# Attention probabilities kept whole: fp32 products of 64 columns in place of split fp32r products of 128

## Chip, cores and metric

One core of a Trainium2 chip runs the whole program in one launch. The metric is the device time of one execution in microseconds; the kernel before took 707.22 us (median of three runs, 707.11 to 707.36).

## The reference, cut to what matters

The work is an attention block with a mask from clusters, then a token and channel mixing by a Fourier transform with an MLP, then a gated convolution block. The change touches only the last product of the attention.

```python
q, k, v: (2, 8, 768, 64)   # batch, heads, tokens, head size
mask   = q_assign[:, :, :, None] == k_assign[:, :, None, :]
scores = scale * q @ k.T ; scores = where(mask, scores, -1e9) - max
attn   = exp(scores) / (sum(exp(scores)) + 1e-9)
out    = attn @ v                       # then mixing and the two MLP blocks
```

All inputs are fp32, so every product is made either of fp32 operands or of operands split into a high and a low fp32r part.

## The kernel before, in words

The 16 heads (8 heads of 2 batches, number n) run one after the other. A head's 768 query tokens are six tiles t of 128. For each tile:

- `scores` (lines 1327, 1328) writes two PSUM banks of 384 keys each, by two fp32r matmuls per bank.
- `minimum` (line 912, VectorE) takes the row minimum; scores are negated, so it is the maximum.
- `exponent` (line 697, ScalarE) writes the unnormalised probabilities `prob` and their row sums.
- `turn` (line 1338, TensorE) transposes the tile's six blocks of 128x128 into banks 4 and 5, three blocks each; `hf` names the half.
- `store_high` (line 708, ScalarE) writes the fp32r high part of a half into `pt_h`, and `store_low` (line 919, VectorE) the rest, PSUM less the high part, into `pt_l`. Each takes both halves of each tile.
- `values` (line 1352) multiplies half a head (a = 0 or 1, three tiles, 384 columns) by v. For each key block j of six it runs two matmuls, on `pt_h` and on `pt_l`, with the 128 weight columns `v_n[s][:, j, :, :]` = 64 of v's high part beside 64 of its low part. Part 0 has j = 0 to 2, part 1 has j = 3 to 5: six matmuls each.
- `store_o`, `fold_o` (lines 717, 1362) and `store_x` (line 996) add the upper and the lower 64 rows of the result, turn it back, and divide by the row sum.

TensorE's order is written out by hand in `step` and `head`: a step is turn half 0, scores two tiles ahead, turn half 1; between steps stand a part of `values`, a `fold_o`, and every second head the cluster products `dots` (line 1282), else `turn_mask`. `dots` makes four fp32 products of 32 weight columns each over 384 moving columns, in the four column groups of the array. ScalarE and VectorE have `step` and `head` lists of their own in the same order. Turn half hf waits for `store_low` of the same half of the tile before, since banks 4 and 5 are single.

GpSimd splits q, k and the first MLP weights, and in `split_v` (lines 520 to 527) v, from `raw_v`, loaded by SyncE's `load_v` (line 397). SyncE's `serve` waits for that split before it loads the next v.

Of the kernel before, what the change touches and what calls it, by code (L numbers as in the profile page):

```python
# [18 lines left out]
P = 128  # L19
# [4 lines left out]
NT = S // P  # L24
# [23 lines left out]
AHEAD = 1  # L48
W1_AHEAD = 2
# [9 lines left out]
def build(nc, q_t, k_t, v, centroids, w1, w2, w_in, conv_w, w_out, seq_tab, fix_tab, chan_tab, constants, out):  # L59
    main = ExitStack()  # L60
    with main:
# [42 lines left out]
        raw_v = sb(att, "raw_v", [NT * D])  # L104
        q1, k1, q2, k2, v_n = [None] * 2, [None] * 2, [None] * 2, [None] * 2, [None] * 2
        for s in range(2):
            q1[s] = sb(att, f"q1_{s}", [S], F32R)
            k1[s] = sb(att, f"k1_{s}", [S], F32R)
            q2[s] = sb(att, f"q2_{s}", [S], F32R)
            k2[s] = sb(att, f"k2_{s}", [S], F32R)  # L110
            v_n[s] = sb(att, f"v_n{s}", [NT, 2, D], F32R)
            if s == 0:
                mask_n = sb(att, "mask_n", [R, 2, 2 * 2, C])
                mask_r = [sb(att, f"mask_r{j}", [R, P], F32R) for j in range(4)]
        prob = [sb(att, f"prob{s}", [NT, P]) for s in range(2)]
        pt_h = [sb(att, f"pt_h{a}", [NT, HALF], F32R) for a in range(2)]
        pt_l = [sb(att, f"pt_l{a}", [NT, HALF], F32R) for a in range(2)]
# [67 lines left out]
        q_loaded, k_loaded, v_loaded = sem("q_loaded"), sem("k_loaded"), sem("v_loaded")  # L185
# [12 lines left out]
        low_ready = sem("low_ready")  # L198
# [14 lines left out]
        high_ready = sem("high_ready")  # L213
# [6 lines left out]
        v_high, v_split = sem("v_high"), sem("v_split")  # L220
# [165 lines left out]
        def _(sp):  # L386
# [9 lines left out]
            def load_v(i, s):  # L396
                sp.dma_start(raw_v[:, :].rearrange("p (a r d) -> p a r d", a=2, r=R),
                             token_view(v, s, i)).then_inc(v_loaded, 16)

            def serve(i, s, loads=True):  # L400
# [25 lines left out]
                if loads:  # L426
                    sp.wait_ge(v_split, n + 1)
                    load_v(ahead, 1 - s)
# [20 lines left out]
            sp.wait_ge(v_split, 1)  # L449
# [39 lines left out]
        def _(pool):  # L489
# [30 lines left out]
            def split_v(n, s):  # L520
                pool.wait_ge(v_loaded, 16 * n + 16)
                if n >= 2:
                    pool.wait_ge(o_ready, AHEAD + 2 * n - 2)
                raw = raw_v[:, :].rearrange("p (n d) -> p n d", d=D)
                high(v_n[s][:, :, 0, :], raw).then_inc(v_high, 1)
                pool.wait_ge(v_high, n + 1)
                low(v_n[s][:, :, 1, :], raw, as_f32(v_n[s][:, :, 0, :])).then_inc(v_split, 1)

# [67 lines left out]
            split_v(0, 0)  # L596
            scale_q(1)

            for n in range(1, NH):
# [15 lines left out]
                split_v(n, n % 2)  # L615
# [47 lines left out]
        def _(act):  # L663
# [38 lines left out]
            def store_high(n, t, hf):  # L702

                g, a = 6 * n + t, t // R
                act.wait_ge(turn_ready, 2 * g + hf + 1)
                if t % R == 0 and hf == 0 and n:
                    act.wait_ge(o_ready, AHEAD + 2 * n + a - 1)
                nc.scalar.activation(  # L708
                    pt_h[a][:, R * hf:R * hf + R, (t % R) * P:(t % R + 1) * P],
                    ps[:, 4 + hf, 0:HALF].rearrange("p (j c) -> p j c", j=R),  # L710
                    ACT.Copy).then_inc(high_ready, 1)
# [7 lines left out]
            def step(n, s, t, more=True):  # L719
                store_high(n, t, 0)  # L720
# [4 lines left out]
                store_high(n, t, 1)  # L725
# [158 lines left out]
        def _(dve):  # L884
# [116 lines left out]
            def step(n, s, t, more=True):  # L1001

                store_low(n, t, 0)
# [4 lines left out]
                store_low(n, t, 1)  # L1008
# [6 lines left out]
            def head(i, s):  # L1015
# [7 lines left out]
                store_low(n, 5, 0)  # L1023
                denominator(n, s, 0)
                minimum(m, 1 - s, 1)
                store_low(n, 5, 1)
                invert(n, 0)
                store_low(m, 0, 0)
                denominator(n, s, 1)
                minimum(m, 1 - s, 2)  # L1030
                store_low(m, 0, 1)
                invert(n, 1)
                store_x(n, s, 0, i)
                store_low(m, 1, 0)
# [3 lines left out]
                store_low(m, 1, 1)  # L1038
                if dotting:
                    hits(u)  # L1040
                store_low(m, 2, 0)
# [3 lines left out]
                store_low(m, 2, 1)  # L1045
# [5 lines left out]
            def last_head(i, s):  # L1051
# [3 lines left out]
                store_low(n, 5, 0)  # L1055
                denominator(n, s, 0)
                store_low(n, 5, 1)
# [205 lines left out]
        def _(pe):  # L1263
# [67 lines left out]
            def turn(n, t, hf):  # L1331
# [3 lines left out]
                if g:  # L1335
                    pe.wait_ge(low_ready, 2 * g - 1 + hf)
# [424 lines left out]
```

## Time and profile before

| what | value |
|---|---|
| median of three runs | 707.22 us |
| the profiled execution, its own time | 707.65 us |
| its span, first to last instruction | 705.8 us |
| TensorE busy | 694.2 us, 98% |
| VectorE, ScalarE, GpSimd busy | 375.7, 309.5, 254.7 us |
| heads, from the first turn to the last values | about 18 to 264 us |

A busy share says that records lie over the time, not that the array streams at its best: matmuls overlap, and a short wait between two of them can be covered by the record of the one before. The chain of work that ended last shows it better. It gives each piece of work the time from the end of the piece before to its own end, so that a late matmul group shows as a longer piece. The view by stretches gives busy times in a part of the span.

### The profile page before, as it was taken

The page shows a single profiled execution, that of the slowest core. Times are in us where ns is not written, and L with a number is a line of the kernel's source. Part 1 is how long each engine was busy: PE and PEld are TensorE (multiplying, and loading weights), DVE is VectorE, ACT ScalarE, POOL GpSimd, SP SyncE. Part 2 cuts the span into 40 slices and gives each one's busy share as a digit, 9 for nine tenths or more (in the row PEclk, how much of TensorE's full clock was granted, in tenths as well). Part 3 has the DMA queues.
Part 4 walks back from the last instruction along what each step waited for, and adds up shares of the span by engine and source line. Part 5 has one row for each costly group of instructions (what it writes and reads, how often), then busy time and mean ns, then how long its engine had stood idle before and what let it go on. Part 6 is the DMA issues. An engine that isn't in the chain of part 4 may idle for free.

```text
span 705.8 us, 10209 instructions
## 1 busy us (share of the span) xinstructions
PE 694.2 (98%) x3810; PEld 607.6 (86%) x3810; DVE 375.7 (53%) x710; ACT 309.5 (44%) x634; POOL 254.7 (36%) x280
## 2 busy tenths in 40 slices
PE   8899999999999999999999999999999999999998
PEld 7699889899999999888888888888888899988876
DVE  4898988979888856953113211131111489933410
ACT  4777777777778851311111111121111377743411
POOL 6756896696499132388600000000050070000000
PEclk7899999999999999999999999999999999999999
DMA  5453424434245021143200000010050520000011
GB/s 170 132 134 103 122 78 130 136 81 114 63 130 162 19 66 33 31 120 107 72 1 0 1 1 0 1 60 1 1 178 1 159 80 1 1 31 30 31 46 45
DMA packets 25921, 47.11 MB, mean 67 GB/s; under 512 B 3728, under 2 KB 10768, under 8 KB 25616
## 3 DMA queue, kind: packets, MB, share of 16 engines
q1 hardware_dynamic: 23392, 38.11, 19.2%
q0 software_dynamic: 2336, 7.95, 3.5%
q8 instruction: 31, 0.51, 0.3%
q10 hardware_dynamic: 144, 0.39, 0.2%
q14 instruction: 18, 0.15, 0.1%
HBM read 36.02 MB, written 3.15 MB: 55 GB/s over the span
## 4 chain that ended last, share of the span: by engine, by line
PE 92%; DVE 6%; ACT 1%; issue 1%; POOL 0%; DVEq 0%; ACTq 0%; POOLq 0%
PE ps L1590 19%; PE ps L1556 19%; PE ps L1352 10%; PE ps L1338 10%; PE ps L1638 9%; PE ps L1652 9%; PE ps L1327 5%; PE ps L1328 5%; PE ps L1362 3%; PE ps L1433 2%; PE ps L1282 1%; PE ps L1403 1%; PE ps L1488 1%; DVE pt_l L919 1%; PE ps L1575 1%
## 5 line engine op out<-in xcount | busy, mean ns | idle before, releaser
L1160 DVE SCALAR_TENSOR_TENSOR hid_l<-ps,hid_h 128x512 fp32r<-128x512 f32 x48 | 33.2, 692 | 197.1 <-ACT hid_h L806 197.1
L806 ACT ACTIVATE hid_h<-ps 128x512 fp32r<-128x512 f32 x48 | 28.8, 599 | 223.6 <-PE ps L1556 223.6
L919 DVE TENSOR_TENSOR pt_l<-ps,pt_h 128x384 fp32r<-128x384 f32 x192 | 106.0, 552 | 36.3 <-ACT pt_h L708 35.9
L708 ACT ACTIVATE pt_h<-ps 128x384 fp32r<-128x384 f32 x192 | 94.6, 494 | 37.0 <-PE ps L1338 36.8
L1338 PE MATMUL ps<-cst,prob 128*128 128x128 f32 x576 | 97.3, 278 | 2.3 <-DVE pt_l L919 1.2
L912 DVE TENSOR_REDUCE row_min<-ps 128x1 f32<-128x768 f32 x96 | 91.2, 950 | 2.3 <-PE ps L1328 2.3
L1338 PEld LDWEIGHTS ps<-cst,prob 128*128 128x128 f32 x576 | 69.3, 142 | 21.9 <-issue 14.3
L697 ACT ACTIVATE prob<-ps,row_min 128x768 f32<-128x768 f32 x96 | 86.5, 901 | 2.4 <-DVE row_min L912 2.4
L1590 PE MATMUL ps<-w_h,hid_h 128*128 128x512 f32 x192 | 76.2, 397 | 0.0
L1590 PE MATMUL ps<-w_h,hid_l 128*128 128x512 f32 x192 | 75.5, 393 | 0.0
L1590 PE MATMUL ps<-w_l,hid_h 128*128 128x512 f32 x192 | 74.7, 389 | 0.0
L1327 PE MATMUL ps<-k,q 80*128 80x384 f32 x192 | 74.2, 386 | 0.3 <-issue 0.3
L1352 PE MATMUL ps<-pt_h,v_n 128*128 128x384 f32 x192 | 69.9, 364 | 0.7 <-DVE x L996 0.7
L1328 PE MATMUL ps<-k,q 128*128 128x384 f32 x192 | 66.5, 346 | 0.0
L1352 PE MATMUL ps<-pt_l,v_n 128*128 128x384 f32 x192 | 64.7, 337 | 0.0
L643 POOL DMA_DIRECT2D in_h<-in_moe_w_in x4 | 2.2, 561 | 162.8 <-PE ps L1556 162.8
L1221 DVE SCALAR_TENSOR_TENSOR gate<-act_s,taps,gate 128x768 f32<-128x768 f32 x32 | 36.0, 1125 | 34.3 <-ACT gate L843 33.8
L1638 PE MATMUL ps<-xt_h,in_h 128*128 128x384 f32 x128 | 43.6, 341 | 0.0
L1590 PEld LDWEIGHTS ps<-w_h,hid_l 128*128 128x128 f32 x192 | 36.0, 188 | 8.5
L1638 PE MATMUL ps<-xt_l,in_h 128*128 128x384 f32 x128 | 43.2, 338 | 0.0
L1638 PE MATMUL ps<-xt_h,in_l 128*128 128x384 f32 x128 | 43.2, 338 | 0.0
L1590 PEld LDWEIGHTS ps<-w_l,hid_h 128*128 128x128 f32 x192 | 36.1, 188 | 7.9
(179 smaller groups left out, 1515.0 us busy)
## 6 DMA issues: line engine op xcount, KB each, us to landing
w_raw<-in_moe_w_ch SPq DMA_DIRECT2D x24, 256.0 KB, 2.5
raw_d<-in_q SPq DMA_DIRECT2D x8, 384.0 KB, 3.3
raw_v<-in_v SPq DMA_DIRECT2D x16, 192.0 KB, 2.5
out<-out_s SPq DMA_DIRECT2D x12, 256.0 KB, 2.0
raw_qk<-in_k SPq DMA_DIRECT2D x15, 192.0 KB, 3.3
raw_qk<-in_q SPq DMA_DIRECT2D x15, 192.0 KB, 3.2
q<-q SPq DMA_DIRECT2D x15, 192.0 KB, 3.9
k<-k SPq DMA_DIRECT2D x15, 192.0 KB, 3.4
```

Source lines behind the costliest of these rows:

```text
L697: nc.scalar.activation(prob[t % 2][:, :, :].rearrange("p (h j) c -> p h (j c)", h=2), ps[:, 2 * (t % 2):2 * (t % 2) + 2, 0:HALF], ACT.Exp, ...
L708: nc.scalar.activation(pt_h[a][:, R * hf:R * hf + R, (t % R) * P:(t % R + 1) * P], ps[:, 4 + hf, 0:HALF].rearrange("p (j c) -> p j c", j=R ...
L912: nc.vector.tensor_reduce(row_min[:, col:col + 1], ps[:, 2 * (t % 2):2 * (t % 2) + 2, 0:HALF], axis=AX.XY, op=ALU.min).then_inc(min_ready, 1)
L919: nc.vector.tensor_tensor(pt_l[a][part], ps[:, 4 + hf, 0:HALF].rearrange("p (j c) -> p j c", j=R), as_f32(pt_h[a][part]), ALU.subtract).th ...
L1327: nc.tensor.matmul(bank, q2[s][0:D + C, cols], k2[s][0:D + C, keys], start=True, stop=False)
L1328: last = nc.tensor.matmul(bank, q1[s][:, cols], k1[s][:, keys], start=False, stop=True)
L1338: last = nc.tensor.transpose(ps[:, 4 + hf, j * P:(j + 1) * P], prob[t % 2][:, R * hf + j, :], ident)
L1352: last = nc.tensor.matmul(ps[:, o_bank(n, a), 0:HALF], v_n[s][:, j, :, :], src[:, j, :], start=j == 0 and src is pt_h[a], stop=j == NT - 1 ...
L1556: last = nc.tensor.matmul(ps[:, hid_bank(blk, f), :], st[:, kt, :], mv[:, kt, :], start=kt == 0 and m == 0, stop=kt == KT - 1 and m == 2)
L1590: last = nc.tensor.matmul(ps[:, 4 + j, :], st[f % 2][:, toks], mv[:, f, :], start=f == 0 and n == 0, stop=f == FT - 1 and n == 2)
L1638: last = nc.tensor.matmul(bank, st[:, kt, cols], mv[:, kt, toks], start=kt == 0 and m == 0, stop=kt == KT - 1 and m == 2)
L1652: last = nc.tensor.matmul(ps[:, 6 + n % 2, :], st[:, f, toks], mv[:, f, :], start=f == 0 and m == 0, stop=f == FT2 - 1 and m == 2)
```

## The change

- `pt_h`, `pt_l` become `pt[n % 2][a]`, one fp32 copy of each turned tile, double over the heads. ScalarE's `store_left` copies the left half (bank 4), VectorE's `store_right` the right one (bank 5): one copy of 128x384 per engine and tile where there were two.
- v isn't split. SyncE loads it straight into one of three fp32 buffers, after the head that used the buffer before has finished its products. GpSimd's `split_v` is gone.
- `values` makes one fp32 product per key block, of 64 weight columns over 384 moving ones. Even j go to array columns and PSUM partitions 0 to 63, odd j to 64 to 127; the fold after it is as before and now adds even and odd blocks. Part 0 has four products, part 1 two.
- TensorE's `step` runs the scores first and then both turn halves; the other engines' lists follow.

```diff
+V_BUFS = 3
-        pt_h = [sb(att, f"pt_h{a}", [NT, HALF], F32R) for a in range(2)]
-        pt_l = [sb(att, f"pt_l{a}", [NT, HALF], F32R) for a in range(2)]
+        pt = [[sb(att, f"pt{par}{a}", [NT, HALF]) for a in range(2)] for par in range(2)]
+        v_n = [sb(att, f"v_n{j}", [NT, D]) for j in range(V_BUFS)]
...
             def load_v(i, s):
-                sp.dma_start(raw_v[:, :].rearrange("p (a r d) -> p a r d", a=2, r=R),
-                             token_view(v, s, i)).then_inc(v_loaded, 16)
+                n = 2 * i + s
+                if n >= V_BUFS:
+                    sp.wait_ge(o_ready, AHEAD + 2 * (n - V_BUFS) + 2)
+                sp.dma_start(v_n[n % V_BUFS][:, :, :].rearrange("p (a r) d -> p a r d", a=2),
+                             token_view(v, s, i)).then_inc(v_loaded[n % V_BUFS], 16)
...
                 if loads:
-                    sp.wait_ge(v_split, n + 1)
                     load_v(ahead, 1 - s)
...
-            def store_high(n, t, hf):
+            def store_left(n, t):
                 g, a = 6 * n + t, t // R
-                act.wait_ge(turn_ready, 2 * g + hf + 1)
-                if t % R == 0 and hf == 0 and n:
-                    act.wait_ge(o_ready, AHEAD + 2 * n + a - 1)
+                act.wait_ge(turn_ready, 2 * g + 1)
+                if t % R == 0 and n >= 2:
+                    act.wait_ge(o_ready, AHEAD + 2 * (n - 2) + a + 1)
                 nc.scalar.activation(
-                    pt_h[a][:, R * hf:R * hf + R, (t % R) * P:(t % R + 1) * P],
-                    ps[:, 4 + hf, 0:HALF].rearrange("p (j c) -> p j c", j=R),
-                    ACT.Copy).then_inc(high_ready, 1)
+                    pt[n % 2][a][:, 0:R, (t % R) * P:(t % R + 1) * P],
+                    ps[:, 4, 0:HALF].rearrange("p (j c) -> p j c", j=R),
+                    ACT.Copy).then_inc(left_stored, 1)
...
             def step(n, s, t, more=True):
-                store_high(n, t, 0)
                 if t < 5:
                     exponent(n, s, t + 1)
                 elif more:
                     exponent(n + 1, 1 - s, 0)
-                store_high(n, t, 1)
+                store_left(n, t)
...
-            def store_low(n, t, hf):
+            def store_right(n, t):
                 g, a = 6 * n + t, t // R
-                dve.wait_ge(high_ready, 2 * g + hf + 1)
-                part = (slice(None), slice(R * hf, R * hf + R), slice((t % R) * P, (t % R + 1) * P))
-                nc.vector.tensor_tensor(pt_l[a][part], ps[:, 4 + hf, 0:HALF].rearrange("p (j c) -> p j c", j=R),
-                                        as_f32(pt_h[a][part]), ALU.subtract).then_inc(low_ready, 1)
+                dve.wait_ge(turn_ready, 2 * g + 2)
+                if t % R == 0 and n >= 2:
+                    dve.wait_ge(o_ready, AHEAD + 2 * (n - 2) + a + 1)
+                nc.vector.tensor_copy(pt[n % 2][a][:, R:2 * R, (t % R) * P:(t % R + 1) * P],
+                                      ps[:, 5, 0:HALF].rearrange("p (j c) -> p j c", j=R)).then_inc(right_stored, 1)
...
                 if g:
-                    pe.wait_ge(low_ready, 2 * g - 1 + hf)
+                    pe.wait_ge((left_stored, right_stored)[hf], g)
...
                 if part == 0:
-                    pe.wait_ge(low_ready, 12 * n + 6 * a + 6)
-                    pe.wait_ge(v_split, n + 1)
+                    for stored in (left_stored, right_stored):
+                        pe.wait_ge(stored, 6 * n + 3 * a + 3)
+                    pe.wait_ge(v_loaded[n % V_BUFS], 16 * (n // V_BUFS + 1))
                     if 2 * n + a:
                         pe.wait_ge(x_stored, AHEAD + 2 * n + a - (o_bank(n, a) == 7))
-                for j in range(R * part, R * part + R):
-                    for src in (pt_h[a], pt_l[a]):
-                        last = nc.tensor.matmul(ps[:, o_bank(n, a), 0:HALF], v_n[s][:, j, :, :], src[:, j, :],
-                                                start=j == 0 and src is pt_h[a],
-                                                stop=j == NT - 1 and src is pt_l[a])
+                for j in ((0, 1, 2, 3), (4, 5))[part]:
+                    at = D * (j % 2)
+                    last = nc.tensor.matmul(ps[at:at + D, o_bank(n, a), 0:HALF], v_n[n % V_BUFS][:, j, :],
+                                            pt[n % 2][a][:, j, :], start=j < 2, stop=j >= NT - 2)
...
             def step(n, s, t):
 
-                turn(n, t, 0)
                 if t < 4:
                     scores(n, s, t + 2)
                 else:
                     scores(n + 1, 1 - s, t - 4)
+                turn(n, t, 0)
                 turn(n, t, 1)
```

## Rows read from the trace of the kernel before

**Rows 1.** The page: busy time by engine, and TensorE's granted clock in 40 slices.
```profile
PE 694.2 (98%) x3810; PEld 607.6 (86%) x3810; DVE 375.7 (53%) x710; ACT 309.5 (44%) x634; POOL 254.7 (36%) x280
...
PEclk7899999999999999999999999999999999999999
```

**Rows 2.** The page: the chain that ended last, by engine and by line.
```profile
PE 92%; DVE 6%; ACT 1%; issue 1%; POOL 0%; DVEq 0%; ACTq 0%; POOLq 0%
PE ps L1590 19%; PE ps L1556 19%; PE ps L1352 10%; PE ps L1338 10%; PE ps L1638 9%; PE ps L1652 9%; PE ps L1327 5%; PE ps L1328 5%; PE ps L1362 3%; PE ps L1433 2%; PE ps L1282 1%; PE ps L1403 1%; PE ps L1488 1%; DVE pt_l L919 1%; PE ps L1575 1%
```

**Rows 3.** Busy time by stretch: length, engines, granted clock, DMA share, GB/s.
```profile
42.00:252.00 210.00, 209.08 (x1428) 191.40 (x1427) 180.86 (x373) 164.72 (x378) 145.12 (x166) 1.00 0.39 104
17.00:42.00 25.00, 23.04 (x144) 18.72 (x137) 21.21 (x42) 19.17 (x44) 16.11 (x17) 0.91 0.43 121
```

**Rows 4.** Groups by line and form, 100 to 180 us: busy, mean ns, idle before.
```profile
L919 DVE TENSOR_TENSOR pt_l<-ps,pt_h 128x384 fp32r<-128x384 f32 x64 | 35.3, 552 | 10.4 <-ACT pt_h L708 10.3
...
L708 ACT ACTIVATE pt_h<-ps 128x384 fp32r<-128x384 f32 x64 | 31.6, 493 | 12.6 <-PE ps L1338 12.6
L912 DVE TENSOR_REDUCE row_min<-ps 128x1 f32<-128x768 f32 x32 | 30.4, 950 | 0.0
L697 ACT ACTIVATE prob<-ps,row_min 128x768 f32<-128x768 f32 x32 | 28.8, 901 | 0.0
...
L697 ACT ACTIVATION_READ_ACCUMULATOR prob<-ps,row_min 128x1 f32 x31 | 6.4, 206 | 0.0
```

**Rows 5.** The chain in order of time, 95.2 to 125.7 us: start, length, what.
```profile
98.00 0.33 PE ps L1338 x3
...
101.47 0.44 PE ps L1338 x3
...
103.99 0.12 issue
104.11 0.52 PE ps L1338 x3
...
105.58 0.21 PE ps L1327
...
106.36 0.52 PE ps L1338 x3
106.89 1.06 PE ps L1352 x6
...
120.38 0.27 PE ps L1327
```

**Rows 6.** The chain in order of time, 229.9 to 258.5 us, heads without dots.
```profile
233.01 0.46 PE ps L1338 x3
```

**Rows 7.** The chain in order of time, 10 to 42 us: dots and the turn behind.
```profile
34.17 0.78 PE ps L1282 x8
34.95 0.48 PE ps L1338 x3
```

**Rows 8.** Line 1282, 124.80 to 125.20 us: ns min/median/max, first and last start.
```profile
L1282 PEld LDWEIGHTS ps<-raw_d,cen_b x8: 106/108/109, 124.9 to 125.0; 128*32 128x32 f32 x8
L1282 PE MATMUL ps<-raw_d,cen_b x4: 510/510/510, 124.9 to 124.9; 128*32 128x384 f32 x4
```

**Rows 9.** The chain in order of time, 10 to 42 us: the first head.
```profile
19.29 0.56 DVE pt_l L919
...
28.14 0.57 DVE pt_l L919
```

**Rows 10.** The chain in order of time, 229.9 to 258.5 us: the last head.
```profile
252.54 0.74 DVE row_min L912
...
254.28 1.31 PE ps L1352 x6
```

**Rows 11.** SyncE's queue, 0 to 262 us: who it waited for, total, times, longest.
```profile
SPq L397 <- POOL v_n L497: 95.6, 15, 9.6
```

More of the change, by code:

```diff
@@ L103, in build @@
         raw_qk = sb(att, "raw_qk", [S])
-        raw_v = sb(att, "raw_v", [NT * D])
-        q1, k1, q2, k2, v_n = [None] * 2, [None] * 2, [None] * 2, [None] * 2, [None] * 2
+        q1, k1, q2, k2 = [None] * 2, [None] * 2, [None] * 2, [None] * 2
         for s in range(2):
@@ L110, in build @@
             k2[s] = sb(att, f"k2_{s}", [S], F32R)
-            v_n[s] = sb(att, f"v_n{s}", [NT, 2, D], F32R)
             if s == 0:
@@ L184, in build @@
         cst_loaded, cen_loaded = sem("cst_loaded"), sem("cen_loaded")
-        q_loaded, k_loaded, v_loaded = sem("q_loaded"), sem("k_loaded"), sem("v_loaded")
+        q_loaded, k_loaded = sem("q_loaded"), sem("k_loaded")
+        v_loaded = [sem(f"v_loaded{j}") for j in range(V_BUFS)]
         q2_copied = [sem(f"q2_copied{s}") for s in range(2)]
@@ L197, in build @@
         min_ready = sem("min_ready")
-        low_ready = sem("low_ready")
+        right_stored = sem("right_stored")
         x_stored = sem("x_stored")
@@ L212, in build @@
         exp_ready = sem("exp_ready")
-        high_ready = sem("high_ready")
+        left_stored = sem("left_stored")
         o_stored = sem("o_stored")
@@ L219, in build @@
         q_split, k_split = sem("q_split"), sem("k_split")
-        v_high, v_split = sem("v_high"), sem("v_split")
         cen_cleared = sem("cen_cleared")
@@ L448, in _ @@
             sp.dma_start(stage[:, 0, 0], w1[0, :, :]).then_inc(w1_raw_loaded[0], 16)
-            sp.wait_ge(v_split, 1)
             load_v(0, 1)
@@ L518, in split_qk @@
                 pool.wait_ge(k_split, n + 1)
[L520 to L527, printed above, removed]
             def split_w1(f):
@@ L595, in _ @@
             pool.wait_ge(k_split, 1)
-            split_v(0, 0)
             scale_q(1)
@@ L614, in _ @@
                     split_w1(n)
-                split_v(n, n % 2)
                 if n in (12, 13):
@@ L1001, in step @@
             def step(n, s, t, more=True):
-                store_low(n, t, 0)
                 if t < 4:
@@ L1007, in step @@
                     minimum(n + 1, 1 - s, t - 4)
-                store_low(n, t, 1)
+                store_right(n, t)
             def z_low_part(b, m):
@@ L1022, in head @@
                 step(n, s, 4)
-                store_low(n, 5, 0)
                 denominator(n, s, 0)
                 minimum(m, 1 - s, 1)
-                store_low(n, 5, 1)
                 invert(n, 0)
-                store_low(m, 0, 0)
+                store_right(n, 5)
                 denominator(n, s, 1)
                 minimum(m, 1 - s, 2)
-                store_low(m, 0, 1)
                 invert(n, 1)
+                store_right(m, 0)
                 store_x(n, s, 0, i)
-                store_low(m, 1, 0)
                 if dotting:
@@ L1037, in head @@
                 minimum(m, 1 - s, 3)
-                store_low(m, 1, 1)
                 if dotting:
                     hits(u)
-                store_low(m, 2, 0)
+                store_right(m, 1)
                 if dotting:
@@ L1044, in head @@
                 minimum(m, 1 - s, 4)
-                store_low(m, 2, 1)
+                store_right(m, 2)
                 if dotting:
@@ L1054, in last_head @@
                 step(n, s, 4, more=False)
-                store_low(n, 5, 0)
                 denominator(n, s, 0)
-                store_low(n, 5, 1)
+                store_right(n, 5)
                 invert(n, 0)
```

## The prediction, as written before the result

> **What bounds the kernel now.** I read first the page's busy times. TensorE has records over 98% of the span, and from slice 3 on its granted clock is at the top of its two levels, 2.4 GHz [rows 1]; no other engine passes 53%. Then the chain of work that ended last: TensorE holds 92% of it, and the edited product, line 1352, holds 10% of the span, as does the turn, line 1338 [rows 2]. The view by stretches says where the change can act. From 42 to 252 us TensorE is covered for 209.1 of 210 us, while VectorE (180.9) and ScalarE (164.7) are busy but not full [rows 3]. So an engine that is relieved gives nothing by being relieved; it gives back only the short waits that it causes on TensorE. What counts is the time that TensorE's own pieces take, plus those waits. Both are read from the chain in order of time, since a piece there runs from the end of the one before to its own end.
>
> **Waits that can go.** A turn half (three transposes) takes 0.33 us where nothing holds it up; in the same two heads others take 0.44, 0.12 + 0.52, and 0.52 [rows 5]. The steps behind them all wait for `store_low` of the tile before, that is for a chain turn, store_high (493 ns), store_low (552 ns) with a minimum of 950 ns or an exponent of 901 ns in between [rows 4]. I added what TensorE's pieces in the 30 us of that double head have over their usual length, without the piece behind dots: 0.11, 0.31 and 0.19 from the rows just named, 0.05 of issue ahead of the last, and seven smaller extras that make 0.67, the first a score matmul of 0.21 and the last one of 0.27 where 0.18 is usual: 1.3 us. Such a double head repeats from 42 to about 206 us, 5.4 times: 7.1 us. In the heads without dots the largest extra is 0.13 [rows 6], and all make about 0.2 us per head, four times: 0.8 us. Together 7.9 us.
>
> After the change ScalarE has per tile 901 + 206 (reading the sum) + 493 = 1.6 us and VectorE 950 + at most 552 = 1.5 us [rows 4], against steps of some 2.5 us (15 us a head, six steps). Turn half 0 of the next tile needs `store_left`, which has the second turn half, the values or fold, and the next scores (four matmuls, 0.7 us) to hide behind, about 1.8 us against 0.6. I take all 7.9 us as gained, and keep a third of it as uncertain.
>
> **The first head.** From 19 to 28.8 us the chain runs over VectorE: minima, cluster steps, and seven `pt_l` pieces of 0.46 to 0.57 us, 3.5 us in all [rows 9]. Four right copies take the place of eight low ones, so about 1.5 us of that chain goes; clock and cluster steps stay (the granted clock is 0.91 from 17 to 42 us [rows 3], and a TensorE kept fuller may hold it up, or the scores ahead of the turns may cost some of it back). I take -1.5, between -2.5 and 0. **The last head.** values waits for `store_x` of the head before, behind a minimum and a low store on VectorE: 1.31 us where six matmuls take 1.06, after 3 us of chain on other engines, the 0.74 us minimum among them [rows 5, 10]. One low store fewer (0.55): -0.6.
>
> **What the products cost.** Before: 1.06 us per part [rows 5], 2.11 per half head. After, nothing here has 64 columns, and the nearest rows are those of dots: four fp32 products of 32 columns over 384, one in each column group. Each makes two passes: the eight matmuls start in two bunches, the first four all at 124.9 us [rows 8], and all eight take 0.78 us [rows 7]. So column groups run side by side, each with its own moving columns. A pass over 384 fp32 columns is 0.33 us, by the three transposes of 128 columns in one 0.33 us turn half [rows 5]; hence dots is two passes, 0.65, and 0.12 us of entry. The turn half behind it takes 0.48 in place of 0.33 [rows 7]: 0.15 us of exit. I read both as what it costs to change between a whole array and column groups, since values and turns change into one another at no such price.
>
> Part 0 has four products, two per group, four passes deep: 0.12 + 4 x 0.325 = 1.42. Part 1 has two passes: 0.78. With two exits 2.50 us against 2.11: +0.39 a half head, 32 times, +12.5. Behind seven parts dots follows, in column groups too, and the last two parts stand together: -1.3. Weights of 64 columns load longer than those of 32 (106 ns [rows 8]), the third and fourth pass of a group need a weight load that dots never shows, and the exit now leads into a score matmul with its 128-column weights: 0 to 0.1 us for each of 63 sections, I take 0.035, +2.3. Sum for the products: **+13.5 us**, from +9 to +18. The streaming alone would have been a gain: six passes are 1.95 us against 2.11. The price is the 63 changes.
>
> On this the Trainium skill says, in "TensorEngine Tiling (Array Packing)", Key Properties, that a change of tiling mode drains the engine, though tiles within one mode run side by side. By that rule, the trace agrees: 0.12 + 0.15 us at dots.
>
> **The rest.** GpSimd loses 16 splits of v; TensorE doesn't wait for GpSimd, so nothing. SyncE waited 95.6 us for them at the v load [rows 11], and now waits there for o of head n - 2, the product that those splits waited for themselves: never later than before, so loads and `load_dots` behind it in the queue come no later. v's bytes and descriptors are the same. Everything after 264 us shifts as a whole.
>
> **Sum.** 707.65 (the profiled execution, 705.8 span and 1.85 around it) + 13.5 - 7.9 - 1.5 - 0.6 = 711.15; the profiled execution is 0.43 above the median, so 710.7 us, 0.5% slower. A measurement here tells about 0.2% (1.4 us) from no change.
>
> **Rivals.**
> 1. *The passes queue up.* Matmuls are issued product by product, first pass, second pass; if a second pass that waits for its own group also holds up the other group, one pass (0.33) is lost in each of 63 sections, +20: 731 us. Against: four first passes at 124.9 us. If the column groups didn't overlap at all, six more passes per half head, 32 x 1.95 = +62: about 773. Rows 7 and 8 speak against both, for 32 columns. The Trainium skill, in "TensorE: Matmul & The Clock Gate", Part 3, says that matmuls start and end strictly in program order. By that rule the first of these would come true; whether the bunches of rows 8 are out of program order the trace can't tell.
> 2. *Changing the groups is cheap* (the other side): the 0.27 us at dots belong to its own waits (mask_stored, raw_d) and not to the array. Then the products cost 12.5 - 63 x 0.27 and the 2.3 less, about -4 and with the waits -14: 693 us. Half that price gives 702. It decides where a change in and out costs under about 0.21 us (0.27 - 3.5/63). For it: dots waits on two semaphores. Against: values and turns wait too and pay nothing, and the turn behind dots pays as well.
> 3. *The waits stay*: `store_left` stands behind the exponent of the next tile; if that is late, the 7.9 us come back in part: 715 to 719.
> 4. *Both sides cancel*: changes at 0.2 us rather than 0.3, 705.8 to 708.6.
>
> **Chances.** Forecast as worked out (708.7 to 715) 0.42; waits stay (715 to 720) 0.10; queued passes 0.08, no overlap 0.02; cancel 0.16; cheap changes 0.22. So slower 0.62, same 0.16, faster 0.22. The range takes the half-price case and most of rival 1's first: 698 to 727; the forecast's own range is 708.7 to 715.
>
> **What would show it.** In the chain from 42 us on: values pieces of about 1.4 (eight matmuls, two per product) and 0.8 us (four); the first piece behind each 0.15 longer; turn halves otherwise all 0.33. Matmul records of 128*64, in bunches of two. VectorE in 42 to 252 us down from 181 to about 135 and ScalarE from 165 to about 123 (14 heads, six stores of 552 or 493 ns fewer each). In the first 30 us the chain leaves VectorE about 1.5 us earlier. Pieces near 1.75 and 1.1 would be rival 1; pieces of 1.3 and 0.65 with no longer follower, rival 2; turn halves over 0.4, rival 3. I am wrong above all if 64 columns behave unlike 32.

## The result and the profile after

The changed kernel took 713.99 us against 707.29 us for the kernel before, both medians: the ratio is 1.008, with an interval of 1.006 to 1.010, so it is slower. One of its six executions took 860.52 us at a mean granted clock of 0.751, where the others have 0.99 or more, and the ratio leaves it out. A second batch of the same kernel gave 711.93 us and 1.006 (1.0045 to 1.0076). The forecast was 710.7, with 708.7 to 715 as its own range, and 698 to 727 with the neighbouring cases in it.

The page of the kernel after, with the busy times of the engines, the granted clock in 40 slices and the chain by engine, which answer to [rows 1] and [rows 2]:

```profile
PE 701.9 (99%) x3810; PEld 568.6 (80%) x3810; DVE 332.8 (47%) x614; ACT 278.4 (39%) x538; POOL 229.5 (32%) x248
...
PEclk9999999999999999999999999999999999999999
...
PE 93%; DVE 5%; ACT 1%; issue 1%; POOL 0%; DVEq 0%; POOLq 0%
```

The view by stretches of the same kernel (length, then PE, PEld, DVE, ACT and POOL busy, granted clock, DMA share, GB/s), against [rows 3]:

```profile
42.00:252.00 210.00, 210.00 (x1394) 152.22 (x1393) 140.75 (x281) 134.47 (x286) 123.66 (x138) 1.00 0.39 104
```

VectorE fell from 180.9 to 140.8 us and ScalarE from 164.7 to 134.5 in the middle stretch, and TensorE's records cover all 210.0 us of it where they covered 209.1. The relief on the other engines is real, but the time as a whole hides what it gave; the run whole_array below tells it apart from what the products cost. The costliest groups on the page, where the two halves of each turned tile now take one copy each, against [rows 4]:

```profile
L1334 PE MATMUL ps<-pt,v_n 128*64 128x384 f32 x384 | 75.8, 503 | 0.3 <-DVE x L983 0.3
...
L697 ACT ACTIVATE pt<-ps 128x384 f32<-128x384 f32 x96 | 47.0, 490 | 52.7 <-PE ps L1319 52.7
...
L908 DVE COPY pt<-ps 128x384 f32<-128x384 f32 x96 | 52.0, 542 | 4.1 <-PE ps L1319 4.1
```

The chain in order of time (start, length, what) from 95 to 128 us, which answers to [rows 5] and [rows 7]. Line 1334 is `values`, 1319 the turn, 1308 and 1309 the scores, 1263 `dots`, 1280 `turn_mask`:

```profile
96.83 0.78 PE ps L1263 x8
97.62 0.37 PE ps L1308
...
98.52 0.66 PE ps L1319 x6
...
101.50 1.44 PE ps L1334 x8
102.94 0.38 PE ps L1308
103.31 0.18 PE ps L1309
...
104.50 0.80 PE ps L1334 x4
...
111.91 0.80 PE ps L1334 x4
112.70 0.48 PE ps L1280 x3
```

Part 0 takes 1.44 us and part 1 0.80. A score matmul takes 0.18 where other scores precede it (0.23 behind a `fold_o`), and 0.37 or 0.38 behind a section in column groups, so the exit is 0.19 to 0.20; into the transposes of `turn_mask` it is 0.48 less 0.33 = 0.15. Both turn halves together take 0.66 = 2 x 0.33: the 0.44, 0.52 and 0.12 + 0.52 of [rows 5] are gone.

### The profile page after: what moved, and what is told of

Read it like the earlier page. It is cut to its first block, busy times and chain, and to the rows that moved or that the text cites. A ratio compares the mean times of both kernels' runs of the same rounds, so it can differ in the third digit from the quotient of the medians.

```text
span 712.0 us, 10028 instructions
## 1 busy us (share of the span) xinstructions
PE 701.9 (99%) x3810; PEld 568.6 (80%) x3810; DVE 332.8 (47%) x614; ACT 278.4 (39%) x538; POOL 229.5 (32%) x248
## 4 chain that ended last, share of the span: by engine, by line
PE 93%; DVE 5%; ACT 1%; issue 1%; POOL 0%; DVEq 0%; POOLq 0%
PE ps L1571 18%; PE ps L1537 18%; PE ps L1334 10%; PE ps L1619 9%; PE ps L1633 9%; PE ps L1319 8%; PE ps L1308 6%; PE ps L1309 5%; PE ps L1343 3%; PE ps L1414 2%; PE ps L1263 1%; PE ps L1384 1%; PE ps L1250 1%; PE ps L1469 1%; PE ps L1280 1%
## 5 line engine op out<-in xcount | busy, mean ns | idle before, releaser
L1319 PE MATMUL ps<-cst,prob 128*128 128x128 f32 x576 | 79.0, 272 | 0.6 <-DVE pt L908 0.6
L1334 PE MATMUL ps<-pt,v_n 128*64 128x384 f32 x384 | 75.8, 503 | 0.3 <-DVE x L983 0.3
L697 ACT ACTIVATE pt<-ps 128x384 f32<-128x384 f32 x96 | 47.0, 490 | 52.7 <-PE ps L1319 52.7
L1308 PEld LDWEIGHTS ps<-k,q 80*128 80x128 f32 x192 | 36.9, 192 | 35.3 <-issue 19.7
L908 DVE COPY pt<-ps 128x384 f32<-128x384 f32 x96 | 52.0, 542 | 4.1 <-PE ps L1319 4.1
```

What stands on the lines that cost most here:

```text
L697: nc.scalar.activation(pt[n % 2][a][:, 0:R, (t % R) * P:(t % R + 1) * P], ps[:, 4, 0:HALF].rearrange("p (j c) -> p j c", j=R), ACT.Copy).t ...
L908: nc.vector.tensor_copy(pt[n % 2][a][:, R:2 * R, (t % R) * P:(t % R + 1) * P], ps[:, 5, 0:HALF].rearrange("p (j c) -> p j c", j=R)).then_i ...
L1308: nc.tensor.matmul(bank, q2[s][0:D + C, cols], k2[s][0:D + C, keys], start=True, stop=False)
L1319: last = nc.tensor.transpose(ps[:, 4 + hf, j * P:(j + 1) * P], prob[t % 2][:, R * hf + j, :], ident)
L1334: last = nc.tensor.matmul(ps[at:at + D, o_bank(n, a), 0:HALF], v_n[n % V_BUFS][:, j, :], pt[n % 2][a][:, j, :], start=j < 2, stop=j >= NT - 2)
```

## Where the difference lies

I cut the trace at the ends of `values` (32 of them, two a head), worked out from the records of its matmuls. The first ends at 34.17 us before and 34.97 after, the 29th at 243.96 and 250.12, the last at 263.9 and 270.18. What follows the last is the same, 441.9 and 441.8 us. So the span's 6.2 us lie in the heads: +0.8 up to the first end, +5.4 over the 28 half heads between (a pair of heads with its `dots` takes 30.93 us where it took 30.25), and +0.1 in the last three.

The first of these has a part that isn't the change's. The chain of the kernel before at the start, with the first cluster products and the first VectorE work behind them:

```profile
5.91 1.54 PE ps L1269 x12
...
7.55 0.37 DVE dot_max L929
```

The same place in the kernel after:

```profile
6.47 5.34 PE ps L1250 x24
...
11.84 0.37 DVE dot_max L916
```

And in the second profile of the kernel after, called after_again below:

```profile
6.38 1.54 PE ps L1250 x12
```

The same code gives 12 matmuls in 1.54 us (0.128 each) once and 24 in 5.34 (0.22 each) the other time. VectorE takes up the last of these products at 9.46 us before, at 11.84 after and at 9.92 in after_again, and the last end of `values` in the two profiles of one kernel is 270.18 and 267.57 us: 2.6 us of the 6.2 are chance.

The times of all executions bear the same sign. In every kernel the executions with a mean granted clock of 0.997 or more are the longest, by about 1 to 3 us over the median of the others, and the three profiles with a mean of 1.000 (after, pool_load, early_turn_first) are the three with the piece of 5.34 us. Of the kernel before, 13 of 63 executions are of this kind; of the kernel after, 3 of the 5 counted in the first batch and 1 of 6 in the second, which is a part of why 713.99 and 711.93 differ. Without them the second batch gives 711.86 against 707.21 us, 4.7 us. So only medians over several executions of the same kind, or the 28 half heads alone, tell small effects apart.

## Experiments

The theory: TensorE's own time for the products grew by the entry into and the exit from column groups, and relief of waits took back part of it. The rivals: the products cost little and something else slowed down (weight loads, the order of the step, GpSimd), or the passes of the two groups hold one another up. Each ratio is against the kernel before on the same chip; not all runs were on one chip.

| kernel | median, us | ratio (interval) | a pair of heads with dots, us |
|---|---|---|---|
| after | 713.99 | 1.008 (1.006 to 1.010) | 30.93 |
| after_again | 711.93 | 1.006 (1.0045 to 1.0076) | 30.93 |
| whole_array | 696.78 | 0.985 (0.983 to 0.986) | 29.07 |
| three_parts | 720.36 | 1.018 (1.017 to 1.020) | 32.15 |
| one_group | 752.91 (one execution) | – | 36.08 |
| groups_apart | 712.56 | 1.007 (1.005 to 1.009) | 30.95 |
| old_order | 712.14 | 1.006 (1.005 to 1.008) | 30.77 |
| before_scores_first | 706.01 | 0.997 (0.996 to 0.999) | 30.03 |
| pool_load | 711.75 | 1.006 (1.004 to 1.007) | 30.92 |
| one_late | 707.75 | 1.001 (1.000 to 1.002) | 30.53 |
| one_early | 704.67 | 0.9965 (0.9952 to 0.9978) | 30.04 |
| late_early | 706.84 | 0.9986 (0.9973 to 0.9999) | 30.39 |
| early_turn_first | 710.51 | 1.0032 (1.0019 to 1.0045) | 30.54 |

**The kernel after once more.** No edit.

> The changed kernel once more, unaltered, for its start. In its first profile the 24 first cluster products (line 1250) took 5.34 us at the lower clock, where the kernel before and four other variants of the changed one took 3.4 us. Theory (the clock's rise falls in or behind them by chance, from execution to execution): this profile may show either length, and the fast times spread over two groups 1 to 2.5 us apart, as 712.98 and 714.03 did. Rival (the change itself makes the start longer): 5.3 us again, and times of 714 alone.

711.93 us, and a start like that of the kernel before: its rows stand above. The pair of heads is the same 30.93 us to the hundredth.

**Products on the whole array.** Stores and order as after, but the copies are stored as fp32r, and the products are fp32r products of 128 weight columns on them. The weights are columns of the probabilities themselves and no longer v, so the output isn't the attention; what is left is the count and the shape of the matmuls of the kernel before.

```diff
-        pt = [[sb(att, f"pt{par}{a}", [NT, HALF]) for a in range(2)] for par in range(2)]
+        pt = [[sb(att, f"pt{par}{a}", [NT, HALF], F32R) for a in range(2)] for par in range(2)]
...
-                for j in ((0, 1, 2, 3), (4, 5))[part]:
-                    at = D * (j % 2)
-                    last = nc.tensor.matmul(ps[at:at + D, ...], v_n[n % V_BUFS][:, j, :], pt[n % 2][a][:, j, :], ...)
+                for j in range(R * part, R * part + R):
+                    for m in range(2):
+                        last = nc.tensor.matmul(ps[:, ...], pt[n % 2][a][:, j, m * P:(m + 1) * P], pt[n % 2][a][:, j, :], ...)
```

> The changed kernel with the product of the kernel before in its place: twelve fp32r matmuls of 128 weight columns per half head (its weights are columns of the probabilities themselves, v is loaded and not used, so the output isn't attention; everything else is as changed). It shows the relief alone, without column groups. Theory (waits worth 8 to 10 us gone, products 15 us dearer): values pieces back at 1.05 us, exits at 0.18, 697 to 699 us, about 1.3% faster than before. Rival (the relief is worth little and the price is small as well): 704 to 707 us.

696.78 us. Its chain from 95 to 128 us:

```profile
97.05 1.06 PE ps L1334 x6
98.11 0.18 PE ps L1308
...
98.82 0.66 PE ps L1319 x6
```

Around `values` there is no entry, no exit, and no turn that waits. This run splits the change in two. From before to whole_array the 28 half heads fall from 209.79 to 201.90 us: the relief alone is worth 7.9 us there, and 10.7 us in the whole (707.46 - 696.78). From whole_array to after they rise to 215.15: the products cost 13.25 us there, and 711.93 - 696.78 = 15.2 us in the whole.

**Three sections in place of two.** The same six products, two in each section, with one more change in and out. The middle section stands between the scores and the two turn halves of the next step (those lines aren't shown).

```diff
-                for j in ((0, 1, 2, 3), (4, 5))[part]:
+                for j in ((0, 1), (2, 3), (4, 5))[part]:
```

> The six products in three parts of two, the middle one between the scores and the turns of the next step: 30 heads' halves get one section more. Theory of the changes: 30 x (one entry and exit, about 0.12 + 0.15 to 0.20) = +8 to +10 us over the changed kernel, 722 to 724 us; each part 0.78 to 0.80 us. Rival (changes cost nothing): 714 us.

720.36 us. Its chain:

```profile
101.36 0.80 PE ps L1334 x4
102.16 0.37 PE ps L1308
...
103.06 0.80 PE ps L1334 x4
103.85 0.80 PE ps L1319 x6
104.66 0.80 PE ps L1334 x4
```

Three pieces of 0.80, where the sections stood as 1.44 and 0.80: 0.16 more for the same passes, and one more exit, 0.15 into the turn (0.80 or 0.81 against 0.66). The pair of heads has four sections more and takes 1.22 us more: **0.305 us for each change in and out**, for the same products. The added change goes out into transposes; those of the kernel after mostly go out into a score matmul, and by the pieces they cost 0.14 + 0.19 = 0.33. An estimate for the whole from 0.305: two of them in 32 half heads are 19.5 us; six passes deep at 0.325 in place of twelve fp32r matmuls of 0.176 give back 32 x (2.11 - 1.95) = 5.1 us.

**One column group.** Products 0 to 3 all go to the lower group, 4 stays there and 5 goes to the upper one. Even and odd sums mix otherwise than in the kernel after, but the fold adds both.

```diff
-                    at = D * (j % 2)
+                    at = D * (j // 5)
...
-                                            pt[n % 2][a][:, j, :], start=j < 2, stop=j >= NT - 2)
+                                            pt[n % 2][a][:, j, :], start=j in (0, 5), stop=j >= NT - 2)
```

> The changed kernel with key blocks 0 to 4 in the lower column group and block 5 alone in the upper one: the four products of the first part queue in one group, eight passes deep. Theory (groups run side by side, a pass is 0.325 us): the first part grows from 1.44 to 2.74 us, the second stays 0.80, 32 x 1.3 = 42 us more, about 754 us. Rival (the pairs were served in turn anyway): no move.

752.91 us in a single execution, 41 us more than after_again; a pair of heads takes 36.08 us where it took 30.93. Its chain has part 0 and part 1 as

```profile
100.88 2.72 PE ps L1334 x8
...
105.17 0.80 PE ps L1334 x4
```

Eight passes one behind another are 8 x 0.325 + 0.12 = 2.72. With two groups they take 1.44 = 4 x 0.325 + 0.14. So 64-column products run side by side in full, each at the speed of one alone; no overlap would cost 1.28 us a half head.

**Products of a group next to each other.**

```diff
-                for j in ((0, 1, 2, 3), (4, 5))[part]:
+                for j in ((0, 2, 1, 3), (4, 5))[part]:
```

> The changed kernel with the four products of the first part in the order 0, 2, 1, 3: two of the lower column group, then two of the upper. If each group takes its matmuls from the queue on its own, however far ahead: pieces stay 1.44 us and the time 713 to 714 us. If a weight load that waits for its own group holds up what is behind it: the upper group starts two passes later, pieces of about 2.0 us, 30 x 0.6 = 18 us more, about 732 us.

712.56 us, and the piece is 1.45 us as against 1.44:

```profile
107.43 1.45 PE ps L1334 x8
```

In this order both products of the lower group are issued before the first of the upper one. If a pass that waits for its own group held up the other group, the piece would be longer. It isn't: in both orders each group runs on by itself, here up to four passes deep. The starts in the kernel after say the same. Line 1334, from 123.85 to 124.0 us (duration min/median/max, first and last start):

```profile
L1334 PE MATMUL ps<-pt,v_n x2: 537/537/537, 123.9 to 123.9; 128*64 128x384 f32 x2
```

Two first passes begin together. If the two passes of a product are issued one behind the other, which the records don't show, the second pass of the first product stands between them in the program. The Trainium skill, in "TensorE: Matmul & The Clock Gate", Part 3, has matmuls starting and ending strictly in program order; here, between two column groups, the measured pieces decide against it.

**The old order of the step, in the new kernel.** The first half of the turn goes ahead of the scores again.

```diff
             def step(n, s, t):
+                turn(n, t, 0)
                 if t < 4:
...
-                turn(n, t, 0)
                 turn(n, t, 1)
```

> The changed kernel with TensorE's step in the order of before: turn half 0, scores, turn half 1. Theory (the single copy, one stage and two engines side by side, is what removed the waits; the order gives little): double heads of 30.9 to 31.4 us, 711 to 715 us. Rival (the scores between a copy and the next turn are what hides the copy): half of the 8 us come back, 716 to 719 us, with turn pieces over 0.33 us.

712.14 us. Its chain:

```profile
100.58 0.48 PE ps L1319 x3
...
112.10 0.62 PE ps L1343 x6
112.72 0.46 PE ps L1319 x3
```

The exit now leads into transposes and costs 0.15, as at `dots` in [rows 7], instead of 0.19; seven of these a pair of heads make 0.28 us. A turn half of 0.46 behind a fold is a small wait that comes back, 0.13 us, and the difference of the two is about what the pair gained (30.93 to 30.77). The order of the step is worth nothing that the median shows.

**The new order in the kernel before.** The other side of the same question: nothing of the change but the order.

> The kernel before with one part of the change alone, the order: TensorE's step runs scores, then both turn halves; VectorE and ScalarE do minimum and exponent first and then both stores of the tile. Products and splits stay. Theory (the waits come of the low store, one more stage behind the high one on a second engine, and VectorE at 86%): the order alone removes at most half of the 8 us of waits, 702 to 708 us. Rival (the order did it all): 698 to 700 us. Second rival: both stores now end later against the next turn, and it gets slower, 710 us or more.

706.01 us, 0.997; the 28 half heads take 208.24 us, 1.5 less than before. In its chain the double store still holds the turn up in places:

```profile
102.62 0.94 PE ps L1338 x6
...
104.95 0.86 PE ps L1338 x6
...
107.56 0.84 PE ps L1338 x6
```

0.28, 0.20 and 0.18 us over the undisturbed 0.66. The order alone takes 0.22 us off a pair of heads; order and single stores together take 1.18 (whole_array). The relief is thus mostly the stores'.

**GpSimd's splits put back.** Per head, the two operations of the size of v's splits run on a buffer of their own.

```diff
+            def split_load(n):
+                high(load_a[:, :, :], load_a[:, :, :]).then_inc(load_high, 1)
+                pool.wait_ge(load_high, n + 2)
+                low(load_a[:, :, :], load_a[:, :, :], load_a[:, :, :]).then_inc(load_low, 1)
+                pool.wait_ge(load_low, n + 1)
```

> The changed kernel with two GpSimd operations of the size of a v split (128x384) put back at the place of each, on a scratch tile, about 1.5 us a head; v itself still goes in unsplit. It tests a term that the prediction put at nothing. Theory: GpSimd is on no path in the heads, 711 to 714 us, as the changed kernel. Rival (the freed GpSimd time had sped the splits of q and k and so the scores): 2 us or more slower, 714 to 718, with score pieces behind k_split waits.

711.75 us, the same as after_again, and the 28 half heads take the same 215.17 us in both. The work that the change takes off GpSimd was worth nothing. SyncE's wait for it [rows 11] isn't put back by this edit.

**All six products in one section, at the place of part 1.** Half of the changes between modes go.

```diff
+                if part == 0:
+                    return
...
-                for j in ((0, 1, 2, 3), (4, 5))[part]:
+                for j in range(NT):
```

> All six products of a half head stand together at the place of the second part: 32 sections of column groups in place of 63. Theory (each change of the array into column groups and back costs about 0.15 + 0.19 us): 31 x 0.34 = 10.5 us less than the changed kernel, about 703 us, faster than the kernel before by some 0.6%; values pieces of 2.09 us, each with a first score matmul of 0.37 behind. Rival (the products themselves are what is dear, changes are not): no move from 713 to 714 us. Second rival (two steps in a row without products between them bring waits back): turns over 0.33 us a half and 706 to 710 us.

707.75 us against the 703 that I had expected; the pair of heads takes 30.53 us. TensorE's timeline (start, duration of the records, instruction) shows a section of full length and a hole ahead of it:

```profile
97.95 0.49 PE L1319 MATMUL ps<-cst,prob 128*128 128x128 f32 x3
98.82 0.52 PE L1319 MATMUL ps<-cst,prob 128*128 128x128 f32 x3 [0.38 <-ACT prob L686]
```

The profile puts the hole down to ScalarE, but the second turn half waits for VectorE's copy of the right half of the tile before, and VectorE's timeline has that copy behind a minimum and a cluster step:

```profile
96.78 0.96 DVE L900 TENSOR_REDUCE row_min<-ps 128x1 f32<-128x768 f32 x1
97.66 0.55 DVE L943 TENSOR_TENSOR hit<-ps,dot_max 128x384 f32<-128x384 f32 x1
98.12 0.55 DVE L908 COPY pt<-ps 128x384 f32<-128x384 f32 x1
```

It ends at 98.67, and 0.15 us later the turn goes on. In the chain this half ends at 99.34 where 97.95 + 0.66 = 98.61 would be due: 0.73 us, once in each pair of heads. Seven times that is 5.1 us, where 4.8 were missing. The section behind it is 2.08 = 0.13 + 6 x 0.325, as the price of a change foretells. Without the products of part 0 between two steps TensorE comes to the second one before VectorE is through. In the kernel after that section covers it: this is the second rival of the expectation.

**All six products at the place of part 0.** The same edit, with part 1 left out.

> The same six products together, at the place of the first part. Theory of the changes: again about 703 us; it stands one step earlier, so that no dots follow it directly, 7 exits of 0.19 us more than the late place: 704 to 705. Rival (products are dear, changes are not): 713 to 714. Second rival (waits come back because two steps follow each other without products, and o must be ready one step sooner): 706 to 710 with turn halves or store_o waits longer.

704.67 us, 0.9965: faster than the kernel before and than the kernel after.

```profile
100.77 0.75 PE ps L1319 x6
...
102.92 0.66 PE ps L1319 x6
103.58 2.09 PE ps L1336 x12
105.66 0.38 PE ps L1308
```

Here no step waits long; steps that follow one another at once pay 0.1 us (0.75 against 0.66). By pieces the section is 2.09 + 0.19 = 2.28 us against 2.11 before: +0.17, 32 times, +5.4. From whole_array's 696.8 that makes 702.2; of the pair of heads, 30.04 - 29.07 - 4 x 0.17 = 0.29 us remain, two turns of 0.75 the larger part of it; seven times that is 2.0, and the sum 704.2, where 704.7 was measured.

**Late for the first half head, early for the second.**

```diff
-                if part == 0:
+                if part == a:
+                    return
+                if True:
```

> One section of six products per half head, the first half's at the late place (just ahead of dots or turn_mask), the second half's at the early one. Theory: the late place's wait of 1.5 us stood ahead of the second half's products (two steps in a row while VectorE does its cluster steps), and dots directly behind column products saves one change out and in, 0.34 us each second head: about 29.7 us per two heads against 30.04, 702 to 703 us. Rival (the two steps in a row ahead of the first half's products bring a wait of the same size): 705 to 708 us.

706.84 us, and 30.39 for the pair of heads where 29.7 was hoped for. The stall stands ahead of the first half's section now, and VectorE is in the chain over some 5 us, with the cluster mask among its work:

```profile
103.67 0.53 DVE mask_n L964 x2
104.20 0.86 DVE row_min L900
...
105.68 0.52 PE ps L1319 x3
```

**one_early with the old order of the step.** I expected 1 to 2 us from the cheaper exit.

```diff
             def step(n, s, t):
+                turn(n, t, 0)
                 if t < 4:
...
-                turn(n, t, 0)
                 turn(n, t, 1)
```

> one_early with the first half of the turn ahead of the scores again, as the kernel before has it. The mode in which a product section ends is then left into transposes, which showed 0.15 us, and not into a score product, which showed 0.18 to 0.20: 0.04 by two to four sections a pair of heads, 15 pairs, is 1 to 2 us less, so 703 to 704.5 against 704.7. Rival: the order of the step hardly matters, as in old_order, and the score product no longer stands between the section and the transposes, so that these wait for VectorE: turn pieces above 0.52 us (x3) or 0.66 (x6) and 705 to 707.

710.51 us, 5.8 more than one_early and beyond even the rival's 707. They ran on two chips, where the medians of the kernel before differ by 0.4 us. The pair of heads is 0.5 us longer. The 28 half heads are 4.2 us longer (213.24 against 209.07), the last three 0.5. The chain shows where in a pair:

```profile
102.57 0.48 PE ps L1319 x3
...
103.80 0.96 DVE row_min L900
104.76 0.48 DVE pt L908
105.37 0.52 PE ps L1319 x3
```

The exit into transposes is 0.15, as expected. The pieces of VectorE are the new thing. A minimum starts when the scores end (103.78), and the copy of the right half behind it ends at 105.24, 1.46 us after those scores. With the scores first, both turn halves and the next scores and another first half (0.66 + 0.72 + 0.33 = 1.71 us) lie between the scores and the second half that needs the copy. Here it is 0.33 less, 1.38, and the half ends at 105.89 where 103.78 + 1.38 + 0.33 = 105.49 would be due: 0.4 us, at 105.37 and again at 120.27. In old_order, where sections stand between most steps, one half of 0.46 is all that shows of it. The remaining 1.1 us of the 5.8 isn't traced. The start of its profile was the slow one (5.34 us for the first cluster products), but seven of the nine executions behind the median were not of this kind, and their median is 710.30.

## Why the prediction was right, step by step

By medians the change costs 4 to 7 us; forecast were 3.5. I compare with after_again, which has the quick first cluster products of the kernel before, and whose last `values` ends 3.7 us later (267.57 against 263.9).

- **Waits in the heads, -7.9.** Measured -7.9 over the 28 half heads, by before against whole_array, which has the new stores and the new order and none of the new products. Adding up TensorE's pieces over their usual length was the right way: it had found 1.3 us in a pair of heads, and 1.18 went. The rest is the new order's own: the score matmul behind a fold takes 0.23 us for 0.18, four times in a pair.
- **First head, -1.5.** The first end of `values` comes 1.8 us earlier in after_again, with +0.33 of dearer products in it (1.44 + 0.19 + 0.80 - 2.10): -2.1. This term hangs on the start as well. The granted clock goes back from 0.50 to 1.00 at 18.3 us in the profile before, at 15.8 in after_again and at about 19.5 in groups_apart, whose first end is at 33.45, only 0.7 us earlier than before: -1.1. And the profile before alone has a second stretch at 0.50, from 25.1 to 28.5 us; the prediction read the 0.91 of [rows 3] as a standing trait of the first head, and it is one profile's. Both figures lie within the bounds, but how much of them is the change no run here settles. **Last head, -0.6.** The last three half heads fell by 0.9 from before to whole_array. The chain on other engines ahead of the late `values` got shorter, from 2.9 to 1.9 us; that piece itself stays at 1.28 us for 1.31 in whole_array, and is 1.51 for a usual 1.44 in the kernel after.
- **Products, +13.5 (+9 to +18).** Measured +14.6: 0.33 in the first half head, 13.25 in the 28, 1.0 in the last three (20.06 against whole_array's 19.06); by the last ends of after_again and whole_array, 267.57 and 252.80, it is 14.8. The steps held one by one: 1.44 for 1.42, 0.80 for 0.78, and 0.12 to 0.15 for the entry, which rows of `dots` with 32 columns had shown. The term that was too small is the one for loads and for the exit into a score matmul: I took 0.035 us a section, and the pieces show 0.02 + 0.04 = 0.06, 63 times. By three_parts a change that goes out into transposes costs 0.305 us, where dots had shown 0.27; into a score matmul it is 0.33, where I had 0.27 + 0.035.
- **Changes that fall together, -1.3.** The prediction doesn't say what it takes as saved where part 1 and `dots` stand together; seven exits of 0.15 and one whole change of 0.27, for the last two parts, would make its 1.3. What is saved is indeed the exit alone: behind part 1 `dots` still takes 0.78 us, as it does behind whole-array work in the kernel before and in whole_array, so going from 64-column groups to 32-column ones costs the entry again. With the exits as measured the saving is 7 x 0.19 + 0.33 = 1.7 us.
- **GpSimd and SyncE, 0.** For GpSimd confirmed by pool_load. SyncE still waits 72.3 us at the v load in the kernel after, now for the products, and the chain by engine above has no DMA in it; no run puts the old wait back.
- **Rival 1, passes queue up.** Refuted: 1.44 against about 1.75, and groups_apart; one_group gives the price of no overlap, 41 us measured where I had worked out 62 (part 1's two products still ran side by side there). Its own 731 us lay outside the 698 to 727 that were said to take in most of it. **Rival 2, cheap changes.** Refuted by three_parts. The Trainium skill says in "TensorEngine Tiling (Array Packing)", Key Properties, that a change of mode drains the engine; the trace agrees, and these runs put the number on it. **Rival 3, waits stay.** Refuted by turns of 0.66. **Rival 4** asked for 0.2 us a change where it is 0.305.
- **The engines' busy times.** VectorE was to fall to about 135 and ScalarE to about 123 us in the middle stretch, and they fell to 140.8 and 134.5. ScalarE's groups in that stretch, of the kernel before and then of the one after, say why:

```profile
L708 ACT ACTIVATE pt_h<-ps 128x384 fp32r<-128x384 f32 x169 | 83.4, 493 | 32.2 <-PE ps L1338 32.2
```

```profile
L697 ACT ACTIVATE pt<-ps 128x384 f32<-128x384 f32 x83 | 40.7, 490 | 48.8 <-PE ps L1319 48.8
```

The sum of the stores' records fell by 42.7 us, as I had counted. But records of one engine overlap when they follow one another at once, and busy time counts the overlap once: ScalarE's groups in that stretch add up to 197.1 us before and 149.6 after, against 164.7 and 134.5 us of busy time. So 30.2 us went with 86 stores, 0.35 each. A count times a mean is an upper bound for what busy time loses. Neither engine sets the pace, so the time is not touched by it.

What chance did: the profiled run shows 713.94 us, 2.3 more than after_again's, and its heads end 2.6 us later, of which the slow cluster products at the start are 1.9. And the forecast of 3.5 stands nearer to the 3.7 than its terms do to theirs: up to the last `values`, whole_array is 11.1 us ahead of the kernel before where 10.0 were forecast, and the products cost 14.8 where 13.5 were. That these two misses cancel is luck; the mechanism is borne out by the pieces.

## What to carry to other kernels

Count the changes between a whole array and column groups before the passes: each change in and out cost 0.305 us here, nearly as much as one pass of 384 fp32 columns (0.325). None of the sections here pays by itself: even six passes in one, 2.28 us with the exit, are dearer than the 2.11 us of the kernel before. The same products in half as many sections turned +0.6% into -0.35% only because the relief is worth 1.5%. A piece of work on the bound engine also hides what the others do meanwhile; before merging or moving one, ask which chain it covers, since the same section gave 704.7 us at one place and 707.8 at the next. VectorE, relieved by 40 us of 180, and ScalarE, by 30 of 165, gave back 7.9 us, and this can be read beforehand as the bound engine's pieces over their usual length.

## What the hardware showed that I had not expected

- The exit from column groups depends on what follows: 0.15 us into transposes, 0.19 to 0.20 into an fp32r score matmul, in every kernel above. Changing between groups of 64 and of 32 columns costs the entry again (0.78 us for `dots` behind part 1).
- Column groups run on independently in both orders tried, products of the two groups by turns or those of one group first (1.44 and 1.45 us).
- At the start of the program the same 24 small matmuls took 5.34 us in one execution and the first 12 of them 1.54 in another, 0.22 against 0.128 us each. That looks like the lower of the two clock levels, 1.2 GHz. In the kernel before the records of these matmuls are 276 ns long while the granted clock reads 1.00, and 401 ns from 8.0 us on, where it reads 0.50. In the slow start all 24 are 401 ns long, but the clock reads 1.00 there too: its first slice is a 9, where the kernel before has a 7 [rows 1]. Score matmuls still take 522 ns at 18 us in that profile and 340 ns from 20.9 us on, so the reading leaves out a stretch at the lower level. A mean granted clock of 0.997 or more is thus the mark of a slow start here. What decides between the two starts, no run here tells.
